# Reordering the hand-over from SW's spreading to the tile loop: product 7 ahead of tile 0's rows, output products cut in two, copies shared, tile 2's first layer moved up

## What is computed

```python
state = gamma * state + k_t v_t^T            # 4 x 8 heads, 768 steps, head size 64
x[t] = scale * q_t state                     # x: 3072 tokens x 512
logits = x @ phi                             # soft MoE: 8 experts of 4 slots
slot_out = per expert: relu(softmax(logits, tokens).T @ x @ w1) @ w2
x2 = softmax(logits, slots) @ slot_out       # 3072 x 512
noisy = x2 @ w_gate + log1p(exp(x2 @ w_noise)) * noise
top2 of 8 experts per token, weights by softmax of the two
out[token] = sum over its two e: weight_e * relu(x2[token] @ moe2_w1[e]) @ moe2_w2[e]
```

## Time and profile before

| what | us |
|---|---|
| median of 3 runs | 548.78 |
| lowest and highest | 547.09, 551.18 |
| the profiled execution | 547.3 |
| its span, first to last instruction | 545.6 |
| mean granted TensorE clock | 0.969 of full |

### The profile page before, as it was taken

The page is one execution under the profiler, slowest core; times in us unless marked ns, Lnnn a source line. Parts: engine busy times, 40 slices in busy tenths (PEclk is TensorE's granted clock), DMA queues, the critical chain, the costliest instruction groups (busy, mean ns, idle before and its releaser), DMA issues.

```text
span 545.6 us, 13537 instructions
## 1 busy us (share of the span) xinstructions
PE 496.7 (91%) x4845; PEld 294.6 (54%) x4846; DVE 277.1 (51%) x449; ACT 185.3 (34%) x345; POOL 257.9 (47%) x216
## 2 busy tenths in 40 slices
PE   4898989997977568799999999999999999999995
PEld 4686777873476344345545455454554545545452
DVE  1775757565411698573564645454646242332422
ACT  0121222222000835773645544536352222322210
POOL 1222221212000016455686868686887766656543
PEclk9999999998997688899999999999999999999998
DMA  7999999988999999415554452123232343333410
GB/s 274 358 353 417 373 379 389 336 337 305 420 424 426 403 414 380 165 51 193 188 191 136 125 179 55 30 52 52 36 59 43 47 57 44 47 50 41 55 24 1
DMA packets 32358, 107.91 MB, mean 198 GB/s; under 512 B 11567, under 2 KB 12831, under 8 KB 27840
## 3 DMA queue, kind: packets, MB, share of 16 engines
q1 hardware_dynamic: 18144, 92.89, 44.0%
q0 software_dynamic: 14176, 14.49, 14.7%
HBM read 93.87 MB, written 29.43 MB: 226 GB/s over the span
## 4 chain that ended last, share of the span: by engine, by line
PE 81%; DMA 7%; DVE 6%; issue 3%; ACT 1%; POOL 1%; SPq 0%; DVEq 0%; POOLq 0%
PE ps L988 51%; PE ps L971 5%; PE ps L655 4%; PE ps L719 4%; DMA late_w1a<-chunks 3%; PE ps L861 3%; PE ps L839 3%; DMA w_region<-chunks 3%; PE ps L695 2%; PE ps L709 2%; PE ps L730 1%; PE ps L669 1%; DMA rec_region<-records,idx 1%; PE ps L751 1%; PE ps L922 1%
## 5 line engine op out<-in xcount | busy, mean ns | idle before, releaser
L988 PE MATMUL ps<-w_region,s_region 128*128 (+1 forms) x1320 | 294.9, 380 | 1.1 <-ACT s_region L1177 1.1
L988 PEld LDWEIGHTS ps<-w_region,s_region 128*128 128x128 f16 x1320 | 127.1, 98 | 144.8 <-issue 2.6
L1607 DVE SCALAR_TENSOR_TENSOR s_region<-ps,s_region 128x1024 f16<-128x1024 f32 x55 | 67.4, 1225 | 147.0 <-ACT s_region L1177 147.0
L1177 ACT ACTIVATE s_region<-ps 128x1024 f16<-128x1024 f32 x55 | 56.3, 1024 | 182.3 <-PE ps L971 182.3
L606 POOL DMA_INDIRECT out<-s_region,rec_region x41 | 55.8, 1361 | 52.7 <-DVE s_region L1636 49.9
L612 POOL DMA_INDIRECT out<-s_region,rec_region x42 | 67.9, 1616 | 15.1 <-issue 12.2
L600 POOL DMA_INDIRECT rec_region<-records,idx x55 | 62.0, 1127 | 24.8 <-issue 16.5
L546 POOL TENSOR_TENSOR s_region<-w_region,s_region 128x512 f32<-128x512 f32 x14 | 14.8, 1058 | 51.4 <-PE ps L730 26.7
L971 PEld LDWEIGHTS ps<-s_region,sw_region 128*128 (+1 forms) x440 | 29.7, 99 | 15.7 <-issue 3.0
L1636 DVE TENSOR_SCALAR s_region<-ps,rec_region,y_scale 128x512 f32<-128x512 f32 x42 | 33.8, 805 | 6.5 <-PE ps L988 4.6
L971 PE MATMUL ps<-s_region,sw_region 128*128 128x128 f16 x440 | 34.5, 222 | 1.9 <-ACT sw_region L1130 1.9
(11 more groups left out here) (248 smaller groups left out, 568.8 us busy)
## 6 DMA issues: line engine op xcount, KB each, us to landing
w_region<-moe_w SPq DMA_DIRECT2D x11, 2048.0 KB, 8.6
w_region<-moe_w SPq DMA_DIRECT2D x15, 1024.0 KB, 9.8
w_region<-chunks SPq DMA_DIRECT2D x26, 512.0 KB, 7.3
w_region<-moe_w SPq DMA_DIRECT2D x24, 512.0 KB, 17.2
s_region<-moe_w SPq DMA_DIRECT2D x4, 2048.0 KB, 15.1
sw_region<-chunks SPq DMA_DIRECT2D x12, 512.0 KB, 7.7
late_w1a<-chunks SPq DMA_DIRECT2D x8, 512.0 KB, 8.6
s_region<-moe_w SPq DMA_DIRECT2D x2, 1024.0 KB, 10.9
```

The lines of the kernel that those rows point to most:

```text
L988: last = nc.tensor.matmul(bank[6 + r], h[:, r, f, :], w2b_parts[:, bass.ds(o, 1), part, f, :].rearrange("p e m -> p (e m)"), start=(first ...
L1177: nc.scalar.activation(h_hi[:, r, :, :].rearrange("p c t -> p (c t)").rearrange("p (a n) -> p a n", a=2), ps[:, 2 + 2 * r:4 + 2 * r, :], A ...
L1607: nc.vector.scalar_tensor_tensor(out=h_lo[:, r, :, :].rearrange("p c t -> p (c t)").rearrange("p (a n) -> p a n", a=2), in0=ps[:, 2 + 2 * ...
```

## The change

PE: product 7 stands ahead of spread 3 and of tile 0's turn; tile 1's turn goes to bank 7 as tile 0's does. out_b(0, 0, 0, True) becomes `first_rows`: 8 matmuls, then spread 4 and 5, four matmuls, spread 6 and 7, four matmuls. Spreads wait for their own low alone and for the copy that last used the bank; the banks are listed in SW_BANKS. Tile 2's hidden_b and tile 3's turn come ahead of tile 1's output products, and the loop begins one step later (k = 1). Copies: DVE has the units 5, 9, 11, 13, 15 and ACT the others. ACT: w2b_sums(EARLY) and w2b_high(EARLY) come behind keep_ct(3), and stage_c(3), h_high(2), keep_ct(3) ahead of them. POOL: three fetches ahead of sw_all_sum instead of six, eight behind; w2b_all_sum(EARLY) behind add_rows(0). DVE: the order is found ahead of sw_scales(0), the tile codes by fewer and smaller operations spread among lows and copies, and w2b_scale_by_sum(EARLY), scale_y(EARLY) and w2b_low(EARLY) stand between h_low(2) and keep_y(1).

```diff
@@ -229,3 +229,3 @@
 tile_no = sb("tile_no", [1, RT], F32)
-tile_cmp = r_region[0:1, 3264:3264 + RT * E].rearrange("p (i e) -> p i e", e=E)
+tile_cmp = r_region[0:1, 3264:3264 + RT * (E - 1)].rearrange("p (i e) -> p i e", e=E - 1)
 tile_e = sb("tile_e", [1, RT], F32)
@@ -237,2 +237,3 @@
 order_expert = sb("order_expert", [1, E], I32)
+order_step = sb("order_step", [1, E - 1], F32)
 first_keys = sb("first_keys", [P, E], F32)
@@ -364,2 +365,5 @@
 SW_GROUPS = ((0, 4), (4, E))
+SW_BANKS = (6, 1, 0, 7, 6, 1, 0, 6, 1, 0, 7, 1, 0, 7, 1, 0)
+SW_BY_DVE = (5, 9, 11, 13, 15)
+SW_BY_ACT = tuple(u for u in range(2 * E) if u not in SW_BY_DVE)
 W2B_SUMS = 2
@@ -398,7 +402,5 @@
-    if unit < E:
-        return sw_act_kept, unit + 1
-    if unit < E + 4:
-        return sw_dve_kept, unit - E + 1
-    return sw_act_kept, unit - 3
+    if unit in SW_BY_DVE:
+        return sw_dve_kept, SW_BY_DVE.index(unit) + 1
+    return sw_act_kept, SW_BY_ACT.index(unit) + 1
@@ -406,3 +408,3 @@
-    return bank[(6, 1, 0)[unit % 3] if unit < E else (7, 1, 0)[(unit - E) % 3]]
+    return bank[SW_BANKS[unit]]
@@ -616,8 +618,7 @@
-    for i in range(DEPTH + 2):
+    for i in range(DEPTH - 1):
         fetch_records(i)
     sw_all_sum(*SW_GROUPS[1])
-    for i in range(DEPTH + 2, 2 * DEPTH + 3):
+    for i in range(DEPTH - 1, 2 * DEPTH + 3):
         fetch_records(i)
-    w2b_all_sum(EARLY)
     for i in range(RT):
@@ -634,2 +635,4 @@
             fetch_records(i + DEPTH + 2)
+        if i == 0:
+            w2b_all_sum(EARLY)
         for o in FIRST:
@@ -902,7 +905,12 @@
     def sw_spread_parts(e):
+        pe.wait_ge(sw_lo_ready, e + 1)
         for half in range(2):
             unit = 2 * e + half
-            if unit >= 3 and unit not in (8, 9, 10):
+            before_it = [u for u in range(unit) if SW_BANKS[u] == SW_BANKS[unit]]
+            if unit == 10:
-                pe.wait_ge(*sw_kept(unit - 3))
+                pe.wait_ge(ct_ready, 2)
+            elif before_it:
+                pe.wait_ge(*sw_kept(before_it[-1]))
             for j in range(2):
@@ -942,3 +950,3 @@
     sw_product(5)
-    pe.wait_ge(sw_lo_ready, 4)
+    pe.wait_ge(idx_ready, 1)
     sw_spread_parts(0)
@@ -947,2 +955,3 @@
     sw_spread_parts(2)
+    sw_product(7)
     sw_spread_parts(3)
@@ -954,5 +963,4 @@
-    pe.wait_ge(idx_ready, 1)
+    pe.wait_ge(*sw_kept(3))
     turn_c(0, 0, 7)
-    sw_product(7)
@@ -994,22 +1002,41 @@
-    hidden_b(0, 0, 0)
-    pe.wait_ge(*sw_kept(6))
-    pe.wait_ge(*sw_kept(7))
-    turn_c(1, 1, 1)
+    def first_rows(part, chunks):
+        for f in chunks:
+            nc.tensor.matmul(bank[6], h_hi[:, 0, f, :], w2b_parts[:, 0, part, f, :],
+                             start=(part == 0 and f == 0), stop=False)
-    out_b(0, 0, 0, True)
-    pe.wait_ge(ct_ready, 2)
-    for e in range(4, E):
-        pe.wait_ge(sw_lo_ready, e + 1)
-        sw_spread_parts(e)
+    hidden_b(0, 0, 0)
+    turn_c(1, 1, 7)
+    pe.wait_ge(*sw_kept(7))
+    pe.wait_ge(w2b_hi_ready, 2)
+    pe.wait_ge(h_hi_ready, 1)
+    first_rows(0, range(FC))
+    sw_spread_parts(4)
+    sw_spread_parts(5)
+    pe.wait_ge(w2b_lo_ready, 1)
+    first_rows(1, range(FC // 2))
+    sw_spread_parts(6)
+    sw_spread_parts(7)
+    first_rows(1, range(FC // 2, FC))
     pe.wait_ge(tile_code_ready, 1)
-    pe.wait_ge(*sw_kept(11))
+    pe.wait_ge(*sw_kept(14))
     pe.wait_ge(*sw_kept(15))
-    kept = pe.alloc_register("kept")
-    pe.reg_load(kept, tile_code[0:1, 1:2])
-    hidden_b(1, 1, expert_of(pe.snap(kept, min_val=0, max_val=E * E - 1)))
+    code = code_of(1)
+    hidden_b(1, 1, expert_of(code))
     turn_c(2, 0, 0)
     out_b(0, 0, 0, False)
-    with pe.Fori(0, (RT - 3) // 2) as k:
+    hidden_b(2, 0, expert_of(code_of(2)))
+    turn_c(3, 1, 1)
+    o = order_of(code)
+    out_b(1, 1, o, True)
+    out_b(1, 1, o, False)
+    kept = pe.alloc_register("kept")
+    pe.reg_load(kept, tile_code[0:1, 2:3])
+    out_b(2, 0, order_of(pe.snap(kept, min_val=0, max_val=E * E - 1)), True)
+    pe.reg_load(kept, tile_code[0:1, 3:4])
+    hidden_b(3, 1, expert_of(pe.snap(kept, min_val=0, max_val=E * E - 1)))
+    turn_c(4, 0, 0)
+    out_b(2, 0, order_of(code_of(2)), False)
+    with pe.Fori(1, (RT - 3) // 2) as k:
         o = order_of(pe.snap(kept, min_val=0, max_val=E * E - 1))
@@ -1159,5 +1186,8 @@
     sw_sums(5)
-    for unit in range(4):
+    for unit in range(3):
         sw_keep(unit)
     sw_sums(6)
+    sw_keep(3)
+    sw_keep(4)
+    sw_sums(7)
@@ -1171,3 +1201,3 @@
         act.wait_ge(ct_turned, i + 1)
-        nc.scalar.activation(ct[:, r, :], bank[7 if isinstance(i, int) and i == 0 else r][:, 0:P // 2].bitcast(F16),
+        nc.scalar.activation(ct[:, r, :], bank[7 if isinstance(i, int) and i < 2 else r][:, 0:P // 2].bitcast(F16),
                              ACT.Copy).then_inc(ct_ready, 1)
@@ -1181,18 +1211,22 @@
     stage_c(0, 0, rec_arrival(0))
-    for unit in range(4, E):
-        sw_keep(unit)
+    sw_keep(6)
     keep_ct(0, 0)
     stage_c(1, 1, rec_arrival(1))
-    sw_sums(7)
-    h_high(0, 0)
-    keep_ct(1, 1)
-    stage_c(2, 0, rec_arrival(2))
+    sw_keep(7)
     act.wait_ge(sw_scale_ready, 2)
-    for e in range(4, E):
+    for e in range(4, 6):
         sw_high(e)
-    w2b_sums(EARLY, junk)
-    for unit in range(E + 4, 2 * E):
+    h_high(0, 0)
+    for e in range(6, E):
+        sw_high(e)
+    keep_ct(1, 1)
+    for unit in range(E, 2 * E, 2):
         sw_keep(unit)
+    stage_c(2, 0, rec_arrival(2))
     h_high(1, 1)
     keep_ct(2, 0)
+    stage_c(3, 1, rec_arrival(3))
+    h_high(2, 0)
+    keep_ct(3, 1)
+    w2b_sums(EARLY, junk)
     w2b_high(EARLY)
@@ -1206,3 +1240,4 @@
     for i in range(3, 3 + UNROLLED):
-        stage_high(i, i % DEPTH, rec_arrival(i))
+        if i > 3:
+            stage_high(i, i % DEPTH, rec_arrival(i))
         for o in FIRST:
@@ -1569,2 +1604,15 @@
                                 ALU.is_equal).then_inc(eq_lo_ready, 1)
+    numbers = count[0:1, 0:E]
+    mask, product = ahead[0:1, :, :], ahead_tiles[0:1, :, :]
+    def by_order(row, values):
+        link(nc.vector.tensor_tensor(product, mask, values.unsqueeze(1).to_broadcast([1, E, E]), ALU.mult))
+        return nc.vector.tensor_reduce(order_e[:, row, :], product, AX_X, ALU.add)
+    link(nc.vector.tensor_reduce(order_e[:, 0, :], ahead[0:1, :, :], AX_X, ALU.add))
+    link(nc.vector.tensor_tensor(mask, order_e[:, 0, :].unsqueeze(1).to_broadcast([1, E, E]),
+                                 numbers.unsqueeze(2).to_broadcast([1, E, E]), ALU.is_equal))
+    link(by_order(1, numbers))
+    nc.vector.tensor_copy(order_expert[:, :], order_e[:, 1, :]).then_inc(order_ready, 1)
     sw_scales(0)
@@ -1580,25 +1628,22 @@
         sw_low(e)
-    numbers = count[0:1, 0:E]
-    link(nc.vector.tensor_reduce(order_e[:, 0, :], ahead[0:1, :, :], AX_X, ALU.add))
-    pairs = ahead_tiles[0:1, :, :]
-    link(nc.vector.tensor_tensor(pairs, order_e[:, 0, :].unsqueeze(1).to_broadcast([1, E, E]),
-                                 numbers.unsqueeze(2).to_broadcast([1, E, E]), ALU.is_equal))
-    link(nc.vector.tensor_tensor(pairs, pairs, numbers.unsqueeze(1).to_broadcast([1, E, E]), ALU.mult))
-    link(nc.vector.tensor_reduce(order_e[:, 1, :], pairs, AX_X, ALU.add))
-    nc.vector.tensor_copy(order_expert[:, :], order_e[:, 1, :]).then_inc(order_ready, 1)
     w2b_low(0)
-    link(nc.vector.tensor_tensor(per_e[0:1, 5, :], per_e[0:1, 3, :], per_e[0:1, 1, :], ALU.add))
-    link(nc.vector.tensor_tensor(tile_cmp[:, :, :], tile_no[:, :].unsqueeze(2).to_broadcast([1, RT, E]),
-                                 per_e[0:1, 5, :].unsqueeze(1).to_broadcast([1, RT, E]), ALU.is_ge))
-    link(nc.vector.tensor_reduce(tile_e[:, :], tile_cmp[:, :, :], AX_X, ALU.add))
-    link(nc.vector.tensor_scalar(tile_e[:, :], tile_e[:, :], float(E - 1), None, ALU.min))
-    nc.vector.tensor_copy(tile_order[:, :], tile_e[:, :])
-    link(nc.vector.tensor_tensor(tile_cmp[:, :, :], tile_e[:, :].unsqueeze(2).to_broadcast([1, RT, E]),
-                                 numbers.unsqueeze(1).to_broadcast([1, RT, E]), ALU.is_equal))
+    sw_keep(5)
+    sw_scales(1)
+    link(by_order(0, per_e[0:1, 3, :]))
+    link(nc.vector.scalar_tensor_tensor(out=order_step[:, :], in0=order_e[:, 1, 1:E], scalar=float(E),
+                                        in1=order_e[:, 1, 0:E - 1], op0=ALU.add, op1=ALU.subtract))
+    for e in range(4, 6):
+        sw_low(e)
+    link(nc.vector.tensor_tensor(tile_cmp[:, :, :], tile_no[:, :].unsqueeze(2).to_broadcast([1, RT, E - 1]),
+                                 order_e[:, 0, 1:E].unsqueeze(1).to_broadcast([1, RT, E - 1]), ALU.is_ge))
+    for e in range(6, E):
+        sw_low(e)
     link(nc.vector.tensor_tensor(tile_cmp[:, :, :], tile_cmp[:, :, :],
-                                 order_e[:, 1, :].unsqueeze(1).to_broadcast([1, RT, E]), ALU.mult))
-    link(nc.vector.tensor_reduce(tile_no[:, :], tile_cmp[:, :, :], AX_X, ALU.add))
```

(30 more changed lines are left out.)

8 lines of the change are left out of this document (4 added, 4 removed).

## The result

| | before | after |
|---|---|---|
| median, us (18 runs of each) | 548.94 | 556.35 |
| ratio after / before | | 1.0128 [1.0099, 1.0157] |
| the profiled execution, us | 547.3 | 556.64 |
| its span, us | 545.6 | 554.9 |
| mean granted clock | 0.969 | 0.966 |

The change costs 1.3%, by the ratio 7.0 us [5.4, 8.6]; the ratio leaves out two of the 18 runs after, which fell into the chip's slower state. The two profiles differ by 9.3 us of span; that of before was 1.6 us under its median, that of after 0.3 over. What follows takes the 9.3 apart.

What follows compares the result with a forecast made beforehand. PE (TensorE) was taken to bound the kernel, any delay of its loop's start delaying the end. Terms 2.8 + 2.8 + 1.6 = +7.2 us take the profiled 547.3 to 554.5; between two bases, 555.2, range 548.5 to 559.5.

Steps and rivals of the forecast that it cites:

- Product 7 earlier: Moving product 7 ahead of spread 3 and the turn gains 0, since its weights land no earlier; start 214.2 to 214.4.
- To tile 0's output products: From product 7 to first_rows, ACT's sums, copies and highs now follow product 7; first_rows begins at 221.9, +2.2 us.
- H: Begin of tile 1's first layer on PE: 231.7 against 228.88, +2.8 us, with first_rows at the low clock.
- My other end: The same steps to tile 1's first layer with first_rows at full clock: begin at 230.0, +1.1 us.
- The loop: ACT's chain of 13.3 us against PE's 9.1 idles PE 4.2 us before turn_c(4); +2.8 us net.
- The clock behind the stall: After the idle before turn_c(4), one low-clock stretch in dense work: +1.6 us, bounds 0 and 3.2.
- POOL: write_rows(0) and add_rows(0) ahead of w2b_all_sum(EARLY): taken as 0, bounds 0 and +1.5 us.
- DVE's second chain: EARLY's scale and w2b_low ahead of keep_y(1), which out_b(3, True) awaits: almost equal to ACT's chain, 0.7 us to spare.
- (1): Stalls stay but PE keeps full clock in first_rows and after turn_c(4): 551.5 to 552.5 us, chance 0.2.
- (2): Everything adds, tile 1's low clock not absorbed and POOL late by 1.5: about 558 us, chance 0.13.
- (3): Faster, ACT's chain before stage_c(4) fitting within PE's 9.1 us: about 546 or 543 us, chance 0.08.
- (4): Stall before turn_c(4) cancelled by an earlier first layer of tile 1: no change, 547 to 550 us, chance 0.12.

Runs made afterwards that it cites:

- e6: e5 with product 7 back behind tile 0's turn, ACT's sums 7 behind unit 7's copy, h_high(0) ahead of the late highs; ratio to before 1.0039.
- e8: The same program as e6, run once more; ratio to the kernel before 1.0078.
- e11: e6 with the register load back behind the two waits and the third w2b's load behind h_high(1); ratio to the kernel before 1.0065.
- e1: Changed kernel with EARLY's sums back ahead of h_high(1), and POOL's reduction and DVE's scale earlier with them; ratio to the kernel before 1.0034.
- e3: e2 with keep_y(1) also put ahead of w2b_low(EARLY) on DVE; ratio to the kernel before 1.0052.
- e4: Changed kernel with only PE's loop order undone, tile 2's first layer again behind tile 1's output products; ratio to the kernel before 1.0182.
- e2: Changed kernel with w2b_sum_part(2, 0) moved from i = 3 to i = 4, behind stage_c(4); ratio to the kernel before 1.0124.
- e5: e1 with tile 1's code loaded to PE's register ahead of first_rows' last four matmuls; ratio to the kernel before 1.0068.
- e7: Kernel before with only the register load of tile 1's code put ahead of spreads 4 to 7; ratio to the kernel before 0.9983.
- e12: Kernel before with the third w2b's load made to wait for h_high(1); ratio to the kernel before 1.0009.

## Why the prediction was right, and which terms were not

The forecast of 555.2 and the measured 556.35 agree, and the mechanism is the one that carries the sum: ACT's chain over EARLY's sums holds turn_c(4), and the clock falls behind it. That the total is so close is partly luck, since a term that was too large and the choice of the base made up for two that were too small. The terms, in its order:

- **Product 7 earlier: 0.** It began at 214.14, held 2.97 us by its weights; 214.2 to 214.4 was said. e6 and e8 to e11 confirm the reason from the other side: put behind the turn it starts at 212.6 to 215.1, and a DMA releases it there too.
- **To tile 0's output products: +2.2.** They began at 221.31 against 219.73, +1.6. ACT went through the order that was worked out, but each small step was a little shorter: unit 7 and its predecessors were done at 219.5 for 220.0, and h_high(0) began at 220.12 for 220.8.
- **H: +2.8.** It was +1.9. The choice of the low clock for first_rows was wrong for this execution (1.89 us for eight, the full clock). My other end, for the full clock, gave H = 230.0, with the last copy done at 229.0. It was done at 229.56, because DVE took it at 228.87, 1.1 us after its matmul had ended at 227.75, and 1.2 us of issue followed where 0.98 was said. In e1, e3 and e4, with the same queue ahead, first_rows took 3.5 us. So both ends of that term exist, and it is a matter of the execution. Counted from product 7's end (217.5 in the forecast) I had H at 12.5 or 14.2 us; it is 12.40 in e2, at full clock and with no copy held up, and 13.55 to 13.75 in e1, e3 and e4 at the low one.
- **The loop: +2.8.** This is the step that was mis-sized. ACT's chain from tile 2's first layer to the record copy took 12.4 us (235.29 to 247.67) for 13.3, the wait for the scale 1.28 for 1.6 and the rest in small parts; so the stall was 3.3 for 4.2. But the turn with its register load behind the stall, 0.9, was left out. Above all I let tile 1's low clock of before vanish into the stall. It stood ahead of the point from which ACT's chain is counted, at tile 2's first layer, and delayed both: 3.88 us from H to it, where 2.3 was said. The stall took up nothing. Counted like this the term is +4.4.
- **The clock behind the stall: +1.6.** It was +2.9, near the upper bound of 3.2: two stretches were granted 0.50 and 0.66, not one.
- **POOL: 0,** as taken, and the short price too. **DVE's second chain** a little behind ACT's: shown by e2, where it surfaced at once.

H was 0.9 too late and the two later terms 1.6 and 1.3 too small, so the profile's sum was 9.2 for 7.2. That the medians lie 7.4 apart, and the forecast next to them, is partly because the profiled execution of before was 1.6 us under its median. The 0.9 that H had too much is itself a difference: the forecast's two ends lie 1.7 apart by the clock of one stretch, which went either way in the profiles here, and the late copy and its register load took 0.8 of it back.

Of the rivals, (1) the kind clock came halfway: first_rows kept its clock, the 24 products did not. The Trainium skill (TensorE: Matmul & The Clock Gate, HAM oscillation) would have first_rows at full clock after a gap of this size; after, e2 and e5 agree (1.89 us behind a gap of 1.74, 1.74 and 1.61), e1, e3 and e4 do not (3.51, 3.48 and 3.53 behind 1.74). The measurements decide: a gap of this size is followed by either level. (2), everything adds, was right that tile 1's low clock comes on top, and wrong on POOL, which waited for ACT. (3), faster, needed ACT's chain below 9.1 us; e1 shows what that takes, and even then H stays late. (4), the stall cancelled by an earlier H, falls with H, which was 1.9 us later than before.

## What to carry to other kernels

When an engine's queue is written out by hand, work moved behind a hand-over does not vanish from it: add up all that stands in that queue between the last thing it can't start earlier and the first thing the bound engine needs, and put the small operation on which the bound engine waits ahead of the big ones. Price a stall of the bound engine with the clock that follows it; here 3.5 us of waiting cost 3.8 us more in register load and low clock. And after taking one wait away, read the next in line first: e2's gain was cut by the chain over keep_y(1), which the prediction had put 0.7 us behind ACT's.

## What the runs showed that I had not expected

**Copies that begin long after their matmul.** In the profiles of before, e1, e2, e3 and e4 a copy that waits for a spread begins some 0.04 us behind the matmul's end. In after and e5 this holds for some of them only, and in e6 and e8 to e11 hardly for any from first_rows on. The times at which the matmuls' semaphore rose, from the raw records, beside the modelled ends of the same matmuls (us; in e11 one of the semaphore's times is missing, and the last four are matched from the end):

```
e1    ends      226.61 226.83 227.25 227.71     semaphore 226.63 226.85 227.26 227.73
after ends      225.94 226.16 226.58 227.75     semaphore 226.66 226.72 227.43 228.85
e11   ends      223.46 223.68 224.94 226.18     semaphore 225.10 226.53 227.96 229.39
```

In e11 the last four rise in steps of 1.43 us, whatever the matmuls do, and the last is 3.2 us late. The profile calls such a wait "remote" or "issue". In after it costs H about 1.1 us, in the family of e6 all that the earlier first_rows had won.

It is not a matter of the changed order. e7 and e12, which have the order of before, show it too: in e7 the matmul that ends at 221.75 raises the semaphore at 223.42. Counted over each trace from the first gather on, no or one signal of TensorE in some 184 came over 0.2 us behind its matmul's modelled end in before and e1 to e4, and 39 to 46 of 169 to 176 did in after and e5 to e12. The two groups divide as the chips do, as far as they are on record: e1 to e4 ran on one chip, e5 to e12 on three others (for the profiles of before and after the chip isn't recorded). The kernel before took 546.89 us on the first of them and 548.2 to 549.5 on the others. So H of after against H of before, and the family of e6 against e1, compare late signals with punctual ones.

The late signals fall into the time in which GpSimd issues its record gathers, one every 1.30 us (1.00 busy and 0.30 of issue) up to 228 or 229 us, and later beside its scatters in the tile loop, where the period stays 5.68 all the same; ahead of the first gather there are none in any profile. But before and e1 to e4 have the same gathers beside punctual semaphores. The cause stays open; moving or halving the gathers was not tried, nor was the kernel of e6 run on the chip of e1.

**The clock of the same stretch differs from execution to execution.** Eight products of 512 columns take 1.89 or 3.5 us with nothing changed ahead of them on any queue. Of these 1.6 us some 1.2 arrive at H (13.55 to 13.75 us from product 7's end against 12.40), more than some of the differences between the profiles compared here.

**A register load behind a wait is not free, and moving it hid little.** It costs 0.65 us behind turn_c(4) in after, and in e5 0.49 us appear where it was moved to. Only 0.4 us of the 1.54 went; in e7 it was 0.75 of 1.89.
